# Three waits on a fused attention and expert kernel's path, and the engine that waits for its last scatter

## The reference

```python
# 1. attention: B=4, H=8, S=576, D=64, causal window of 64 keys
scores = where(mask, q @ k.T / 8, -1e9); attn = softmax(scores)
x = (attn @ v) as rows                      # (2304, 512)
# 2. gated product
h = ((x @ w1) * (x @ w2)) @ w3              # 512 -> 1024 -> 1024
x = h @ w_out                               # (2304, 512)
# 3. eight experts, one per row
logits = x @ w_gate; e = argmax(logits)
p = softmax(logits)[e]; g = sigmoid(x @ w_output_gate)[e]
out[row] = p * g * (relu(x @ w1[e]) @ w2[e])
```

## Time and profile before

| | |
|---|---|
| Time, median of 3 runs | 736.43 us (735.5, 736.43, 736.5) |
| The profiled execution | 736.11 us |
| Its span, first to last instruction | 734.4 us |
| Mean granted TensorE clock | 0.995 |
| TensorE busy | 709.5 us, 97%, 5139 matmuls |
| VectorE, ScalarE, GpSimd busy | 329.8, 298.3, 120.5 us |
| DMA | 80.14 MB, mean 109 GB/s |
| Fold of the weights | up to 85.7 us |
| Chunks 0 to 5 | 85.7 to 449.0 us |
| Slots | 449.0 us to the end |

### The profile page before, as it was taken

How to read it: one execution, slowest core, us unless ns; L and a number is a source line. 1 busy time by engine, 2 the same in 40 slices (tenths; PEclk the granted TensorE clock), 3 DMA queues, 4 the chain that set the end, 5 groups by cost and what they waited for, 6 DMA issues and landing times.

```text
span 734.4 us, 15150 instructions
## 1 busy us (share of the span) xinstructions
PE 709.5 (97%) x5139; PEld 646.4 (88%) x5140; DVE 329.8 (45%) x667; ACT 298.3 (41%) x721; POOL 120.5 (16%) x191
## 2 busy tenths in 40 slices
PE   5999999999999999999999999999999999999994
PEld 5899999999999989999999999878888888888883
DVE  3477554512135524452221568755456544652210
ACT  4477454522135434553211253444455535542211
POOL 6012011200011121111000001222222222222111
PEclk9999999999999999999999999999999999999997
DMA  9596111320012241203301033756266644411100
GB/s 294 181 317 221 47 51 52 102 87 1 15 51 59 65 130 38 79 23 131 142 1 44 1 105 132 245 172 221 83 218 193 230 148 163 147 42 36 38 33 29
DMA packets 48063, 80.14 MB, mean 109 GB/s; under 512 B 5325, under 2 KB 29901, under 8 KB 48016
## 3 DMA queue, kind: packets, MB, share of 16 engines
q1 hardware_dynamic: 42976, 64.01, 27.1%
q0 software_dynamic: 5040, 15.47, 6.1%
HBM read 70.03 MB, written 10.49 MB: 110 GB/s over the span
## 4 chain that ended last, share of the span: by engine, by line
PE 93%; DMA 2%; DVE 2%; ACT 1%; issue 1%; POOL 0%; DVEq 0%; SPq 0%; ACTq 0%; POOLq 0%
PE bank L459 28%; PE bank L461 26%; PE bank L460 26%; PE bank L533 3%; PE bank L661 3%; PE bank L511 2%; PE bank L523 2%; PE bank L639 1%; DMA wo<-in_w_out 1%; DMA w3r<-in_w3T 1%; PE bank L471 1%; PE bank L621 1%; DVE wbuf L981 0%; PE bank L497 0%; PE bank L493 0%
## 5 line engine op out<-in xcount | busy, mean ns | idle before, releaser
L459 PE MATMUL bank<-Wh,abh 128*128 128x272 f32 (+1 forms) x288 | 84.0, 292 | 0.0
L461 PE MATMUL bank<-Wh,abl 128*128 128x272 f32 (+1 forms) x288 | 82.1, 285 | 0.0
L460 PE MATMUL bank<-Wl,abh 128*128 128x272 f32 (+1 forms) x288 | 81.8, 284 | 0.0
L981 DVE TENSOR_TENSOR wbuf<-raw,wbuf 128x1024 f32 (+1 forms) x64 | 75.3, 1222 | 13.7 <-ACT wbuf L786 13.5
L721 ACT ACTIVATE prob<-prob,nmx 128x128 f32<-128x128 f32 x144 | 56.3, 392 | 60.7 <-DVE nmx L898 60.7
L1280 POOL TENSOR_TENSOR prob<-prob,rec 128x384 f32<-128x384 f32 x48 | 39.8, 829 | 212.6 <-DVE rec L908 208.7
L459 PE MATMUL bank<-wbuf,hTh 128*128 (+1 forms) x176 | 70.7, 402 | 1.4 <-DVE hTl L1163 1.4
L1163 DVE TENSOR_TENSOR hTl<-bank,hTh 128x512 fp32r<-128x512 f32 x44 | 28.4, 686 | 96.6 <-ACT hTh L824 95.6
L459 PE MATMUL bank<-wbuf,xsTh 128*128 (+1 forms) x176 | 70.4, 400 | 0.2 <-DVE xsTl L1021 0.2
L461 PE MATMUL bank<-wbuf,hTl 128*128 (+1 forms) x176 | 68.8, 391 | 0.0
L461 PE MATMUL bank<-wbuf,xsTl 128*128 (+1 forms) x176 | 68.6, 390 | 0.0
(11 more groups left out here) (198 smaller groups left out, 1499.0 us busy)
## 6 DMA issues: line engine op xcount, KB each, us to landing
raw<-in_expert_w SPq DMA_DIRECT2D x64, 512.0 KB, 4.3
qT<-in_qT SPq DMA_DIRECT2D x24, 192.0 KB, 2.9
kT<-in_kT SPq DMA_DIRECT2D x24, 192.0 KB, 3.4
x_rows<-x_sb POOLq DMA_DIRECT2D x18, 256.0 KB, 2.3
w3r<-in_w3T SPq DMA_DIRECT2D x8, 512.0 KB, 3.8
wo<-in_w_out SPq DMA_DIRECT2D x8, 256.0 KB, 7.2
woT<-in_w_outT SPq DMA_DIRECT2D x4, 512.0 KB, 7.4
vA<-in_v SPq DMA_DIRECT2D x16, 128.0 KB, 2.1
```

What stands on the lines that cost most here:

```text
L459: pe.matmul(dst, lh, rh, start=first, stop=False)
L460: pe.matmul(dst, lh, rl, start=False, stop=False)
L461: return pe.matmul(dst, ll, rh, start=False, stop=last)
L981: dve.tensor_tensor(wbuf[:, bass.ds(wcol(e, part, 1, c * PC), PC)], raw[part * NP1 + c][:, :], f32(wbuf[:, bass.ds(wcol(e, part, 0, c * PC ...
```

## The change

Four edits, each on every engine that it concerns.

1. The last value product (step 13 of the fold and of a chunk with attention) is issued inside the step's own product, behind j or f = 2, which is nine of its 24 matmuls.
2. Banks 0 to 3 rotate by the running chunk `cc` instead of the place `c`. A chunk starts on other banks than the last row tiles used, so its first wait is for fewer copies, at c = 0 too; the special bank of the final row tile goes, and with it its wait; the first expert product waits for `xA_ok`, NT.
3. Expert 1's part 1: ScalarE splits three pieces ahead of `relu(1)` and one behind it; VectorE one ahead of `relu(1)` and three behind `xs_out(2)`. TensorE's hidden(1) and x_transposes(2) move from behind f = 5 to behind f = 6 of project(0).
4. The last scatter reports to a semaphore of its own, for which SyncE waits; GpSimd does not. Ahead of the scatter before the last, GpSimd runs `drain()`. The last scaling reports to a semaphore of its own too.

```diff
@@ sync
                     sp.wait_ge(ew_lo[c // NP1], e * NP1 + (c % NP1 + 1 - NP1))
                     load_piece(e, c)
+            sp.wait_ge(y_last_out, 16)
@@ both rotations
-        def hidden_bank(c, f, m):
-            return bank[(2 * (c + f) + m) % 4]
-        def row_bank(c, i, final):
-            return bank[3] if final and i == 2 * CT - 1 else bank[(2 * c + i) % 4]
+        def hidden_bank(cc, f, m):
+            return bank[(2 * (cc + f) + m) % 4]
+        def row_bank(cc, i):
+            return bank[(2 * cc + i) % 4]
@@ tensor: W_half
-            def W_half(it, n, g1_tile=None):
+            def W_half(it, n, g1_tile=None, between=None):
...
                         mm = product3(dst, wh, wl, oh_j, ol_j, j == 0, j == KF - 1)
+                        if between and j == 2:
+                            between()
...
-                fold_step(attend, attend_end, i, lambda: W_half(...))
+                if i < len(w_order) - 1:
+                    fold_step(attend, attend_end, i, lambda: W_half(...))
+                else:
+                    W_half(it, n, between=lambda: attend_end(0, NSTEP - 1, 0))
@@ tensor: chunk
-                pe.wait_ge(xA_ok, cc * CT + (1 if c == 0 else 1 - 2))
+                pe.wait_ge(xA_ok, max(cc * CT - 1, 1))
...
-                        if f == 1 and c > 0:
+                        if f == 1 and cc > 0:
                             pe.wait_ge(xA_ok, cc * CT + 1)
...
-                    if final and i == 2 * CT - 1:
-                        pe.wait_ge(xA_ok, cc * CT + 2)
...
+                        if between and f == 2:
+                            between()
...
-                    around(attend, attend_end, b, KF + i, parity, lambda: row_tile(i, n, tt))
+                    if b is not None and KF + i == NSTEP - 1:
+                        row_tile(i, n, tt, lambda: attend_end(b, NSTEP - 1, parity))
+                    else:
+                        around(attend, attend_end, b, KF + i, parity, lambda: row_tile(i, n, tt))
@@ tensor: slots
-                if f == KF - 3:
+                if f == KF - 2:
                     hidden(1, 0)
                     x_transposes(2)
...
             pe.wait_ge(xB_ok, NT + 1)
+            pe.wait_ge(xA_ok, NT)
             hidden(0, 0, slot_ids)
@@ scalar
                 if tail == 2:
-                    return y_scaled(s, 1)
+                    act.wait_ge(y_done, s + 2)
+                    act.wait_ge(y_free, s + 1)
+                    act.activation(y_sb[:, :], bank[6][:, :], ...).then_inc(y_last, 1)
+                    return
...
             xs_out(1)
+            act.wait_ge(tab_ok, 1)
+            for c in range(NP1 - 1):
+                split_hi(1, 1, c)
             relu(1)
+            split_hi(1, 1, NP1 - 1)
             xs_out(2)
             act.wait_ge(scale_ok, 1)
             y_scaled(0)
-            act.wait_ge(tab_ok, 1)
-            for c in range(NP1):
-                split_hi(1, 1, c)
@@ vector
             for p in range(NP1):
                 split_lo(1, 0, p)
+            split_lo(1, 1, 0)
             relu(1)
             xs_out(2)
-            for p in range(NP1):
+            for p in range(1, NP1):
                 split_lo(1, 1, p)
@@ gpsimd: body(s, tail)
+                if tail == 1:
+                    pool.drain()
                 pool.tensor_copy(sidc[:, 0:1], sid[:, bass.ds(s, 1)]).then_inc(pool_c, 1)
...
-                scatter(s)
                 if tail == 2:
                     pool.wait_ge(xs_in, s * 16 + 32)
+                    pool.wait_ge(y_last, 1)
+                    scatter(y_last_out)
+                else:
+                    pool.wait_ge(y_ok, s + 2)
+                    scatter(y_out)
+                    pool.wait_ge(y_out, s * 16 + 16)
+                    pool.sem_inc(y_free, 1)
```

More of the change, by code:

```diff
@@ L238, in build @@
         y_done, y_ok, y_out, y_free, turn = sem("y_done"), sem("y_ok"), sem("y_out"), sem("y_free"), sem("turn")
+        y_last, y_last_out = sem("y_last"), sem("y_last_out")
         f32 = lambda ap: ap.bitcast(F32)
@@ L541, in _ @@
                     pe.wait_ge(const_ok, 1)
-                fold_step(attend, attend_end, i, lambda: W_half(it, n, (i - 1) * (KF // 2) if 1 <= i <= 2 else None))
+                if i < len(w_order) - 1:
+                    fold_step(attend, attend_end, i, lambda: W_half(it, n, (i - 1) * (KF // 2) if 1 <= i <= 2 else None))
+                else:
+                    W_half(it, n, between=lambda: attend_end(0, NSTEP - 1, 0))
             def chunk(cc, c, batches, b, parity, final):
@@ L561, in hidden_tile, with row_tile @@
                             xc = slice(kt * SUPER + c * CH, kt * SUPER + (c + 1) * CH)
-                            mm = product3(hidden_bank(c, f, m)[:, 0:CH], wh[:, ws], wl[:, ws], xTh[:, xc], xTl[:, xc],
+                            mm = product3(hidden_bank(cc, f, m)[:, 0:CH], wh[:, ws], wl[:, ws], xTh[:, xc], xTl[:, xc],
                                           kt == 0, kt == KD - 1)
                         mm.then_inc(done, 1)
-                def row_tile(i, n, tt):
+                def row_tile(i, n, tt, between=None):
                     if i == 0:
@@ L579, in row_tile @@
                         ws = slice(f * WXC + first, f * WXC + end)
-                        mm = product3(row_bank(c, i, final)[:, 0:end - first], abh[:, ts], abl[:, ts], Wh[:, ws], Wl[:, ws],
+                        mm = product3(row_bank(cc, i)[:, 0:end - first], abh[:, ts], abl[:, ts], Wh[:, ws], Wl[:, ws],
                                       f == 0, f == KF - 1)
+                        if between and f == 2:
+                            between()
                     mm.then_inc((xA_done, xB_done)[n], 1)
@@ L791, in hidden_tile @@
                     act.wait_ge(a_done, cc * KF + (f + 1))
-                    act.activation(a_sb[f % 2][:, :], hidden_bank(c, f, 0)[:, 0:CH], ACT.Copy).then_inc(a_ok, 1)
+                    act.activation(a_sb[f % 2][:, :], hidden_bank(cc, f, 0)[:, 0:CH], ACT.Copy).then_inc(a_ok, 1)
                     act.wait_ge(ab_ok, cc * KF + (f + 1))
@@ L799, in row_tile @@
                         act.wait_ge(x_free, cc + 1)
-                        act.activation(x_sb[tt][:, 0:HALF], row_bank(c, i, final)[:, 0:HALF], ACT.Copy).then_inc(xA_ok, 1)
+                        act.activation(x_sb[tt][:, 0:HALF], row_bank(cc, i)[:, 0:HALF], ACT.Copy).then_inc(xA_ok, 1)
                 for f in range(KF):
@@ L824, in hT_out, with y_scaled @@
                     act.activation(hTh[last][:, n * 512:(n + 1) * 512], bank[3 + n][:, :], ACT.Copy).then_inc(hT_hi, 1)
-            def y_scaled(s, last=0):
+            def y_scaled(s):
                 act.wait_ge(y_done, s + 2)
                 act.wait_ge(y_free, s + 1)
-                act.activation(y_sb[:, :], bank[5 + last][:, :], ACT.Copy, scale=ssc[:, bass.ds(s, 1)]).then_inc(y_ok, 1)
+                act.activation(y_sb[:, :], bank[5][:, :], ACT.Copy, scale=ssc[:, bass.ds(s, 1)]).then_inc(y_ok, 1)
             def body(s, tail=0):
                 if tail == 2:
-                    return y_scaled(s, 1)
+                    act.wait_ge(y_done, s + 2)
+                    act.wait_ge(y_free, s + 1)
+                    act.activation(y_sb[:, :], bank[6][:, :], ACT.Copy, scale=ssc[:, bass.ds(s, 1)]).then_inc(y_last, 1)
+                    return
                 e1, e2 = next_experts(act, s)
@@ L989, in hidden_tile @@
                     dve.wait_ge(a_ok, cc * KF + (f + 1))
-                    dve.tensor_tensor(ab_f[f % 2][:, :], hidden_bank(c, f, 1)[:, 0:CH], a_sb[f % 2][:, :], ALU.mult).then_inc(ab_ok, 1)
+                    dve.tensor_tensor(ab_f[f % 2][:, :], hidden_bank(cc, f, 1)[:, 0:CH], a_sb[f % 2][:, :], ALU.mult).then_inc(ab_ok, 1)
                     dve.wait_ge(ab_hi, cc * KF + (f + 1))
@@ L998, in row_tile @@
                         dve.wait_ge(x_free, cc + 1)
-                        dve.tensor_copy(x_sb[tt][:, HALF:DM], row_bank(c, i, final)[:, 0:HALF])
-                        dve.tensor_copy(L[:, bass.ds(cc * (CT * LG) + tt * LG, LG)], row_bank(c, i, final)[:, HALF:HALF + LG]).then_inc(xB_ok, 1)
+                        dve.tensor_copy(x_sb[tt][:, HALF:DM], row_bank(cc, i)[:, 0:HALF])
+                        dve.tensor_copy(L[:, bass.ds(cc * (CT * LG) + tt * LG, LG)], row_bank(cc, i)[:, HALF:HALF + LG]).then_inc(xB_ok, 1)
                 for f in range(KF):
@@ L1309, in _, with scatter @@
             for_chunks(chunk)
-            def scatter(s):
-                pool.wait_ge(y_ok, s + 2)
+            def scatter(out_ok):
                 pool.sem_inc(turn, 1)
                 pool.indirect_dma_start(out=out, out_offset=bass.IndirectOffsetOnAxis(ap=sidc[:, 0:1], axis=0),
-                                        in_=y_sb[:, :], in_offset=None, bounds_check=last_row, oob_is_err=False).then_inc(y_out, 16)
-                pool.wait_ge(y_out, s * 16 + 16)
-                pool.sem_inc(y_free, 1)
```

(1 more changed line is left out.)

## The result

| | before | changed |
|---|---|---|
| Time, median of the runs | 735.59 us (6 runs, 735.14 to 736.5) | 724.28 us (6 runs, 723.47 to 726.28) |
| Ratio | | 0.985, 95% interval 0.983 to 0.986 |
| The profiled execution | 736.11 us | 726.28 us |
| Its span | 734.4 us | 724.5 us |

What follows compares the result with a forecast made beforehand. TensorE, with work in 709.5 of 734.4 us, was taken as the bound, so gains lay in its waits and the time after its last product. 3.5 + 0.7 + 1.9 + 5.4 = 11.5 gave 724.9 us, range 723.9 to 730.4.

Steps and rivals of the forecast that it cites:

- Part 1: Fold and three attention chunks: last value product inside the step's own product removes four xTl waits, 4 x 0.88 = 3.5 us.
- Covered: Next chunk's wait for the later last xTl: there by 342.4, while the matmuls left run to about 343.4.
- Part 2: Border of chunks 2 and 3: rotating PSUM banks by running chunk removes the wait for a row-tile copy, 0.7 us.
- Part 3: Start of the slots: earlier splits of the second expert bring the projection of slot 1 from 480.09 to 478.2, 1.9 us.
- The new wait of about 0.2: Before slot 2's hidden product: TensorE would newly wait about 0.2 us for xsTl.
- Part 4: Kernel's end: early GpSimd drain and SyncE's wait for the last scatter take the closing drain off, 5.4 us.
- The choice between 0.18 and 5.22: Closing GpSimd drain: bounds in us for its length after two DMAs; the short one was taken.
- The sign that I had named: Closing rows: GpSimd shows two drains, one of 5 us near 707 and a short last one.
- A: Kernel's end: last drain still 5.22 us but starting at 726.93, gaining 2.1 there; 728.2 us, chance 0.22.
- B: Kernel's end: drain waits for the landing, then takes its 5.22, gaining nothing there; 730.3 us, chance 0.13.
- C: Middle of the kernel: only half the gain comes, 3 of 6.1 us; 728.0 us, chance 0.08.
- D: Before the last scatters: an early drain over 6.5 us delays them; slower, 737.9 us at 17.3, chance 0.03.

Runs made afterwards that it cites:

- run 10: Changed kernel with the last low part of w1 made ahead of the last xTl on VectorE in the fold; 725.39 us, ratio 0.986.
- run 8: Changed kernel with the bank rotation by running chunk undone (banks by place in the group again); 725.30 us in one run.
- run 9: Changed kernel with the new order of expert 1's splits and of the second hidden product undone; 727.11 us, ratio 0.988.
- run 5: Kernel before with only the early GpSimd drain and SyncE's wait for the last scatter added; 730.26 us, ratio 0.992.
- run 2: Changed kernel, early drain kept, but GpSimd and not SyncE waits for the last scatter; 726.12 us, ratio 0.986.
- run 3: Changed kernel with two more GpSimd drains, one behind the chunks and one directly behind the early drain; 726.41 us in one run.
- run 1: Changed kernel without the early drain, SyncE still waiting for the last scatter; 728.90 us, ratio 0.990.
- run 4: Changed kernel with one more GpSimd drain directly behind the scatter before the last, while that is in flight; 725.68 us in one run.

## Why the prediction was right, and where it was off

The time came out 0.6 under the forecast, inside its own range of 723.9 to 725.9. The sum was 11.5; the stretches give 10.9 and the medians 11.3, and the kernel before ran at 735.59 in the longer series, 0.8 under the 736.43 that I had started from. So some luck is in how close it came: the gain was 0.2 to 0.6 short of the sum, and the start was 0.8 too high, which works the other way. By steps:

**Part 1** was said to give 4 x 0.88 = 3.5. It gave 3 x 0.81 in the chunks and 0.54 in the fold: 3.0. Two terms were off. A switch costs on both sides: the value product starts 0.21 behind the matmul before it (270.46 to 270.67, where the pitch is 0.12), besides the 0.10 behind it that I had counted; so 0.81 in place of 0.88. And in the fold I looked at what is late next for xTl alone. Behind that xTl VectorE had the last split of w1 queued, for which chunk 0 waits; run 10 shows it, 0.25 us (behind nine matmuls the chunks had 0.28 of cover where I had worked out 0.20). The sentence "Covered" was true of the chunks, where no weight is split, and not of the fold.

**Part 2**: 0.7 said, 0.70 measured in the table (1.51 less 0.81) and in run 8. Its price in chunk 5, costed at nothing, is nothing: chunks 4 and 5 did not change.

**Part 3**: 1.9 said, 1.90 in the trace, 1.86 undone in run 9. The new wait of about 0.2 before the hidden product of slot 2 is there, 0.26. In the traces of the experiments the projection of slot 1 often runs 0.1 to 0.3 later than in the changed kernel's, with hTl ready at the same place; I did not find out why. One term was wrong without harm: I let hTl start 2.2 behind the start of the last split, since it does before. It started 1.1 behind it, as soon as the splits were through (469.32 + 3.48 and 472.73), so the cover was 1.6 and not 0.7.

**Part 4**: 5.4 said, 5.36 measured, 5.4 alone in run 5. The choice between 0.18 and 5.22 was a guess that a drain goes by the DMAs behind it, and the runs bear it out: 82 to 87 ns per DMA. The old trace held one point of it, 5.22 for 63 DMAs, and the count of DMAs stood in the program. The sign that I had named, a short last drain, misses what happens: the last drain is 3.05 long, since it starts before the landing and waits for it. What counts is that it ends 0.13 behind the landing; its own work is 0.22 (run 2). The rule of the Trainium skill, page "VectorE: DVE Perf Modes", section "The DRAIN you can't avoid" (drains of pre- and postamble constant at about 12 ns, on all five engines), holds here for SyncE's closing drain, 7 ns, and not for GpSimd's, 0.22 to 6.44 us. In the changed kernel the closing drains of VectorE (0.84 us), ScalarE (0.70) and TensorE (4.25) are longer too; each begins while its engine is still at its last work.

**The rivals.** A (fixed price) fell in runs 2 and 3, though its number was what SyncE's wait is worth without the early drain (2.0, run 1). B (the closing drain follows the landing with all its work) would have needed the drain of run 1 to begin at the landing; it began its work at the issue's end. C (half of the middle) fell by the table: 5.5 of 6.1. D (the early drain delays the last scatters) had its cover as worked out: of 6.5 the drain took 5.06, and 1.4 were left. It ended at 713.0, the copy of the row numbers was through at 713.7, and y was there at 715.1.

The range reached up to 730.4 for A and B alone. The trace before could not exclude them, since it has one drain with DMAs behind it and not two.

## What to carry to other kernels

When TensorE is 97% busy, look for the end of the program and for the single gaps, each by what ends it, and read what is queued behind the instruction that you make later: here VectorE's split behind xTl. A wait of an engine on a short chain goes away when independent matmuls of the next tile are put in front of it, and the length of the chain says how many: for 1.48 us nine were enough, three left 0.37 us of idle. Before the end of a kernel with many GpSimd DMAs, let GpSimd drain early, in a stretch where it is idle: the closing drain then has only the last few to pay for, and can hide behind the last landing.

## What the runs showed of the hardware

- A GpSimd DRAIN took 46 ns with no DMA since the last one, and 82 to 87 ns more for each (2, 19, 42, 61 and 63 DMAs of 128 rows of 2 KB), although all had landed before it began. The drain at the start of the program took 183 ns, with no DMA before it. I had expected at most that it falls with the count, not a straight line with nearly no offset.
- It does this work while a later scatter is in flight (5.23 us behind the end of the last scatter instruction, run 1), and it does not end before the last landing (0.09 and 0.13 us behind it, run 4 and the changed kernel).
- A switch of TensorE from products of 256 columns to a value product cost 0.09 us, and the switch back 0.10, beyond the pitch of 0.12 (270.46 to 270.67 in the changed kernel, 341.32 to 341.54 before).
